# Seventeen instead of nine products of the identity with itself ahead of the first expert slot

## The chip, the cores and the metric

One core of one Trainium2 chip runs the whole program. The metric is the device time of one execution in microseconds (us), as the median of several runs. The kernel before takes 744.62 us (three runs, 742.53 to 746.62).

## The reference

The program computes three stages after one another, for a batch of 4 sequences of 576 tokens.

1. Attention with 8 heads of 64 columns, causal, with a bias that is made from a running sum of `s`.
2. A layer of 8 experts (512 to 1024 to 512 columns). Each token goes to one expert. The expert is the largest of 8 gate logits, or the expert of the token before where a local gate is high. The token's row is `relu(x @ w1[e]) @ w2[e]`, weighted by the softmax of the gate at `e`.
3. A dense layer: `h = relu(x @ w_in)`, a convolution of three taps along the tokens, a sigmoid gate, and `(h * gate) @ w_out`.

```python
for b in range(B):
    for s in range(S):
        fresh_e = argmax(logits[b, s])
        e = fresh_e if (s == 0 or local_gate[b, s] < 0.5) else prev_e
        h = maximum(x[b, s] @ w1[e], 0.0)
        out[b, s] = p[e] * (h @ w2[e])
```

## The kernel before, in words

The kernel is written by hand, engine by engine; the order of each engine's instructions is the order of the code, and semaphores join them. TensorE's program is attention, then `tensor_route`, `tensor_experts` and `tensor_block`. Nothing plans or reorders the work.

**Routing** (`tensor_route`, L1007 to L1038). VectorE finds each token's expert and its place in a list sorted by expert. The list is cut in 25 slots of 128 tokens, each slot belonging to one expert. TensorE helps with transposes, counts and sums. Between its waits it runs `keep_running` (L25 to L28): products of the 128x128 identity with itself, written to a PSUM bank that nobody reads. Each call of `matmul` there with float32 operands shows in the profile as two weight loads and two MATMUL rows, so nine products are 18 pairs. The last sum of routing gives the tokens of slots 8 to 24 (L1028, second part). Then comes the transpose of the convolution's weights (L1037), then nine products (L1038, shown as L28). After them begins `tensor_experts`.

**Experts** (`tensor_experts`, L1325 on). TensorE first waits for `slot_ready`, which VectorE gives with `slot_i` (L1141), the small table that says which half of the weight ring a slot uses and how many weight pieces must be there. `weights_of` reads two of its values into TensorE's registers (L1347 and L1348). Then `turn_first_x` (L1335 to L1340) waits for slot 0's tokens, which POOL's indirect DMA gathers from `x_rows` into `x_slots` (L1179), and turns them with four transposes. Two more products follow (L1411, shown as L28). VectorE takes the turned tokens to SBUF as a high and a low part (L1454, L1456). `hidden(0, (0,))` is 12 matmuls (L1365) for the first half of the hidden row. Then come `turn_x(1)` (L1331), the second half of `hidden(0)`, `turn_h(0)` (L1404), `turn_x(2)`, `hidden(1)`, `output(0)` (L1382), `turn_h(1)`, and so on. After slot 2 the pattern per slot is four transposes of tokens, 24 matmuls of L1365 and 24 of L1382.

**The other engines there.** VectorE, in order: the moves of slot 0's tokens, two low parts of expert 1's second matrix (L1530, semaphore `second_low`), the move of slot 1 (L1462, L1464), the moves of slot 0's hidden row (L1505, L1509), the tokens' weights (L1167 to L1174), and the two halves of `relu(1)` (L1496). POOL gathers slots 0 to 7, waits for `second_low`, writes `counted` (L1312), and gathers slots 8 to 24. ScalarE does the relu of slot 0 (L1296). SyncE's queue has nothing to issue there until VectorE hands over the first output row (L1260).

Of the kernel before, what the change touches and what calls it, by code (L numbers as in the profile page):

```python
# [24 lines left out]
def keep_running(nc, bank, identity, times):  # L25

    for _ in range(times):
        nc.tensor.matmul(bank[:, 0:P], identity[:, :], identity[:, :], start=True, stop=True)  # L28
# [744 lines left out]
def mixture(nc, ctx, sems, region, identity, attend, x_rows, y_sorted, w_gate, w_local, w1, w2, w_in, conv_w, w_out, out, h_turn):  # L773
# [89 lines left out]
    wide_bank = [sems.enter_context(nc.psum_tensor(f"wide_bank{n}", [P, 2, 512], F32)) for n in range(2)]  # L863
# [143 lines left out]
    def tensor_route(pe):  # L1007
        keep_running(nc, bank[1], identity, 9)
        pe.wait_ge(code_ready, 2)
        nc.tensor.transpose(wide_bank[0][0:T, 0, 0:P], small["rank_code"][:, :], identity[:, :]).then_inc(code_turned, 1)  # L1010
        keep_running(nc, bank[1], identity, 4)
        pe.wait_ge(seq_ready, 1)
        nc.tensor.matmul(bank[0][:, T:2 * T], expert_seq[:, P - 1:P].to_broadcast([T, P]), identity[0:T, 0:T], start=True, stop=True)
        nc.tensor.transpose(bank[0][:, 0:T], expert_seq[:, :], identity[0:T, 0:T]).then_inc(expert_turned, 1)
        flat_oh = oh[:, :, :].rearrange("p e t -> p (e t)")
        keep_running(nc, bank[1], identity, 4)
        pe.wait_ge(onehot_ready, 1)
        nc.tensor.matmul(wide_bank[1][:, 1, 0:E * T], all_ones[:, :], flat_oh, start=True, stop=True).then_inc(ranked, 1)
        nc.tensor.matmul(wide_bank[1][:, 0, 0:E * T], tri_less[:, :], flat_oh, start=True, stop=True).then_inc(ranked, 1)
        keep_running(nc, bank[1], identity, 15)  # L1020
        for part, slots in enumerate(SLOT_PARTS):
            pe.wait_ge(slot_tokens_ready, part + 1)
            for t in range(T):
                if t in BY_VECTOR:
                    pe.wait_ge(row_ready, t + 1)
                else:
                    pe.wait_ge(last_rows_ready, (t - BY_SCALAR[0]) // 3 + 1)
                last = nc.tensor.matmul((bank[1], row_bank[1])[part][:, 0:slots.stop - slots.start], row_is[:, t, :], slot_token[:, t, slots],  # L1028
                                        start=t == 0, stop=t == T - 1)

                if part == 0 and t % 3 == 1 and t < T - 1:
                    keep_running(nc, wide_bank[1][:, 0, :], identity, 1)
            last.then_inc(tokens_summed, 1)
            if part == 0:
                keep_running(nc, wide_bank[1][:, 0, :], identity, 6)
        pe.wait_ge(conv_loaded, 16)
        nc.tensor.transpose(row_bank[0][:, 0:K * KF], conv_nat[:, :], identity[0:K * KF, 0:K * KF]).then_inc(conv_turned, 1)  # L1037
        keep_running(nc, wide_bank[1][:, 0, :], identity, 9)  # L1038

    CHOICES = (slice(0, T - TB), slice(T - TB, T))  # L1040
    choice_steps = [0]
# [757 lines left out]
    def scalar_block(act):  # L1799
# [85 lines left out]
        for n in range(2):  # L1885
            act.wait_ge(out_stored[n], 16 * (NT // 2))

    return att, dict(sync=((sync_early, sync_between), sync_route, sync_experts), pool=(pool_early, pool_route, pool_experts, pool_block, first_low),
                tensor=(tensor_route, tensor_experts, tensor_block), vector=(vector_early, vector_route, vector_experts, vector_block, lambda dve: vector_choice(dve, 0)),
                scalar=(scalar_route, scalar_experts, scalar_block, first_high, load_gates))  # L1890

# [82 lines left out]
```

## Time and profile before

| what | us |
|---|---|
| median of three runs | 744.62 |
| profiled execution, whole | 744.3 |
| its span, first to last instruction | 742.6 |
| TensorE busy in the span | 720.5 (97%) |
| mean granted TensorE clock | 0.988 of full speed |

The span leaves out 1.7 us that lie around it. The granted clock has two levels in these profiles: 1.00 is 2.4 GHz and 0.50 is 1.2 GHz; a number between them is a stretch that holds both.

### The profile page before, as it was taken

The page shows a single profiled execution, that of the slowest core. Times are in us where ns is not written, and L with a number is a line of the kernel's source. Part 1 is how long each engine was busy: PE and PEld are TensorE (multiplying, and loading weights), DVE is VectorE, ACT ScalarE, POOL GpSimd, SP SyncE. Part 2 cuts the span into 40 slices and gives each one's busy share as a digit, 9 for nine tenths or more (in the row PEclk, how much of TensorE's full clock was granted, in tenths as well). Part 3 has the DMA queues.
Part 4 walks back from the last instruction along what each step waited for, and adds up shares of the span by engine and source line. Part 5 has one row for each costly group of instructions (what it writes and reads, how often), then busy time and mean ns, then how long its engine had stood idle before and what let it go on. Part 6 is the DMA issues. An engine that isn't in the chain of part 4 may idle for free.

```text
span 742.6 us, 13519 instructions
## 1 busy us (share of the span) xinstructions
PE 720.5 (97%) x4227; PEld 591.8 (80%) x4227; DVE 458.7 (62%) x1088; ACT 316.1 (43%) x634; POOL 328.4 (44%) x442
## 2 busy tenths in 40 slices
PE   8999999999979599999999999999999999999998
PEld 6676767767678487888888888888899889889986
DVE  5777778778766355566575665666399445536610
ACT  5777878778430022221412223020488335436620
POOL 8759888898236334644637647240521100000000
PEclk9999999999999799999999999999999999999999
DMA  8988888784075548786768877641421110000011
GB/s 177 217 213 227 207 224 229 210 206 134 17 216 159 137 164 273 252 271 232 256 210 300 255 241 254 220 138 44 142 64 30 43 36 15 30 30 14 29 43 56
DMA packets 114966, 115.35 MB, mean 155 GB/s; under 512 B 63804, under 2 KB 84052, under 8 KB 114900
## 3 DMA queue, kind: packets, MB, share of 16 engines
q1 hardware_dynamic: 94372, 68.54, 32.5%
q10 hardware_dynamic: 17056, 34.69, 14.2%
q0 software_dynamic: 3472, 11.28, 5.6%
q8 instruction: 38, 0.62, 0.3%
q14 instruction: 28, 0.23, 0.1%
HBM read 87.14 MB, written 27.34 MB: 154 GB/s over the span
## 4 chain that ended last, share of the span: by engine, by line
PE 67%; DVE 2%; another core or an unknown queue 2%; issue 1%; DMA 1%; ACT 0%; DVEq 0%; POOLq 0%; ACTq 0%
PE wide_bank L1365 18%; PE wide_bank L1694 14%; PE row_bank L1733 13%; PE row_bank L1382 9%; PE bank L1382 9%; PE bank L1331 1%; PE bank L1663 1%; DMA x_slots<-x_rows,token_of 1%; PE wide_bank L1404 0%; PE bank L1683 0%; PE wide_bank L28 0%; PE bank L1340 0%; PE row_bank L1683 0%; DVE y_sb L1524 0%
## 5 line engine op out<-in xcount | busy, mean ns | idle before, releaser
L914 POOL TENSOR_TENSOR ring<-raw_w,ring 128x2048 fp32r<-128x2048 f32 x28 | 128.7, 4619 | 117.2 <-ACT ring L904 117.2
L904 ACT ACTIVATE ring<-raw_w 128x2048 fp32r<-128x2048 f32 x30 | 55.8, 1908 | 209.3 <-DMA raw_w<-in_moe_w_dram 174.7
L1694 PE MATMUL wide_bank<-x_tr,ring 128*128 128x288 f32 x768 | 107.7, 297 | 0.0
L1694 PEld LDWEIGHTS wide_bank<-x_tr,ring 128*128 128x128 f32 x768 | 103.2, 188 | 0.9
L1733 PE MATMUL row_bank<-ring,g_tr 128*128 128x512 f32 x432 | 100.2, 390 | 0.0
L690 ACT ACTIVATE prob<-score,row_min 128x128 f32<-128x128 f32 (+2 forms) x144 | 83.4, 580 | 38.5 <-PE turn_ps L362 25.6
L1733 PEld LDWEIGHTS row_bank<-ring,g_tr 128*128 128x128 f32 x432 | 80.4, 188 | 16.2
L1785 DVE SCALAR_TENSOR_TENSOR conv<-h_pad,conv_col,conv 128x576 f32<-128x576 f32 x64 | 52.3, 817 | 53.8 <-ACT conv L1846 52.5
L252 POOL TENSOR_SCALAR bias<-ncum_row,cum_col 128x128 f32<-128x128 f32 (+3 forms) x128 | 66.8, 532 | 36.4 <-DVE row_min L551 33.4
L551 DVE CUSTOM_DVE_ANT_0 score<-score_ps,bias 128x128 f32<-128x128 f32 (+2 forms) x144 | 69.2, 514 | 19.9 <-issue 13.6
L1365 PE MATMUL wide_bank<-ring,xs_tr 128*128 x312 | 78.0, 406 | 3.3 <-DVE xs_tr L1456 1.8
L1382 PE MATMUL row_bank<-ring,h_tr 128*128 x312 | 73.4, 390 | 0.1
L1365 PEld LDWEIGHTS wide_bank<-ring,xs_tr 128*128 128x128 f32 x312 | 59.7, 195 | 16.6 <-issue 4.1
L1382 PEld LDWEIGHTS row_bank<-ring,h_tr 128*128 128x128 f32 x312 | 58.4, 188 | 12.9 <-issue 0.9
L1365 PE MATMUL wide_bank<-ring,xs_other 128*128 x288 | 68.5, 393 | 0.0
L1365 PEld LDWEIGHTS wide_bank<-ring,xs_other 128*128 128x128 f32 x288 | 53.2, 188 | 10.6
L1636 POOL DMA_INDIRECT y_tok<-y_sorted,place_i x20 | 20.2, 1008 | 77.2 <-PE bank L1663 46.7
L362 PE MATMUL turn_ps<-identity,prob 128*128 128x128 f32 x320 | 50.1, 279 | 1.0 <-ACT rest_tr L708 0.6
L362 PEld LDWEIGHTS turn_ps<-identity,prob 128*128 128x128 f32 x320 | 36.4, 141 | 11.6 <-issue 5.0
L322 PE MATMUL score_ps<-k_tr,q_tr 64*128 64x128 f32 (+3 forms) x256 | 44.9, 469 | 0.1
L1382 PE MATMUL bank<-ring,h_tr_other 128*128 x192 | 44.8, 389 | 0.0
L1837 ACT ACTIVATE h_pad<-wide_bank 128x576 f32<-128x576 f32 x32 | 20.9, 653 | 55.7 <-PE wide_bank L1694 55.4
(254 smaller groups left out, 1127.7 us busy)
## 6 DMA issues: line engine op xcount, KB each, us to landing
raw_w<-in_moe_w_dram ACTq DMA_DIRECT2D x12, 2048.0 KB, 11.2
x_slots<-h_turn SPq DMA_DIRECT2D x84, 128.0 KB, 2.9
ncum_row<-cum_rows SPq DMA_DIRECT2D x15, 512.0 KB, 4.9
y_sorted<-y_sb SPq DMA_DIRECT2D x26, 256.0 KB, 3.0
raw_w<-in_moe_w_dram SPq DMA_DIRECT2D x12, 512.0 KB, 4.4
h_turn<-h_sb SPq DMA_DIRECT2D x11, 512.0 KB, 5.3
h_turn<-x_slots SPq DMA_DIRECT2D x10, 512.0 KB, 7.2
ncum_tail<-cum_rows SPq DMA_DIRECT2D x32, 144.0 KB, 4.4
```

The costliest lines, as they stand in the source:

```text
L252: return nc.gpsimd.tensor_scalar(out, row, col, 1.0, ALU.add, ALU.mult)
L322: nc.tensor.matmul(out[:, hh, 0:(i + 1) * P], q_tr[u][at, i * P:(i + 1) * P], k_tr[u][at, 0:(i + 1) * P], start=True, stop=True).then_inc( ...
L362: last = nc.tensor.transpose(bank[:, at + j * P:at + (j + 1) * P], prob[unit(p, n) % 4][:, j * P:(j + 1) * P], identity[:, :])
L551: nc.vector.tensor_tensor_reduce(out=o, in0=a, in1=b, scale=1.0, scalar=3.0e38, op0=ALU.add, op1=ALU.min, accum_out=row_min[:, at % 4:at % ...
L690: nc.scalar.activation(prob[at % 4][:, 0:w], score[at % 3][:, 0:w], ACT.Exp, bias=row_min[:, at % 4:at % 4 + 1], scale=-1.0, accum_out=row ...
L904: nc.scalar.activation(high, whole, ACT.Copy).then_inc(high_ready, 1)
L914: nc.gpsimd.tensor_tensor(low, whole, high.bitcast(F32), ALU.subtract).then_inc(low_ready, 1)
L1365: last = nc.tensor.matmul(h_bank[:, half, :], xs_both[s % 2][:, a, kb, :], ring[:, bass.ds(n, 1), b, at:at + FH].rearrange("p a c -> p (a ...
L1382: last = nc.tensor.matmul(y_banks[s % 2][:, :], ht_of(s)[:, a, kb, :], ring[:, bass.ds(n, 1), 2 + b, kb * D:(kb + 1) * D].rearrange("p a c ...
L1694: last = nc.tensor.matmul(wide_bank[j % 2][:, half, 0:HALF], ring[:, 0, w, col:col + P], x2_tr[:, x, kb, at:at + HALF], start=kb == 0 and ...
L1733: last = nc.tensor.matmul(row_bank[outs % 2][:, :], g_tr[:, a, kb, lo:hi], ring[:, 0, 2 + w, kb * D:(kb + 1) * D], start=kb == 0 and (a, w ...
L1785: ins = V.scalar_tensor_tensor(c[:, :], h[:, k:k + S], conv_col[:, k * KF + f:k * KF + f + 1], c[:, :], ALU.mult, ALU.add)
```

## The change

One number: the last call of `keep_running` in `tensor_route` makes seventeen products in place of nine. It writes to the same PSUM bank, waits for nothing and gives no semaphore.

```diff
         pe.wait_ge(conv_loaded, 16)
         nc.tensor.transpose(row_bank[0][:, 0:K * KF], conv_nat[:, :], identity[0:K * KF, 0:K * KF]).then_inc(conv_turned, 1)
-        keep_running(nc, wide_bank[1][:, 0, :], identity, 9)
+        keep_running(nc, wide_bank[1][:, 0, :], identity, 17)
```

## Rows read from the trace of the kernel before

**Rows 1.** The page: busy time, clock in 40 slices, shares of the last chain.
```profile
PE 720.5 (97%) x4227; PEld 591.8 (80%) x4227; DVE 458.7 (62%) x1088; ACT 316.1 (43%) x634; POOL 328.4 (44%) x442
...
PEclk9999999999999799999999999999999999999999
...
PE 67%; DVE 2%; another core or an unknown queue 2%; issue 1%; DMA 1%; ACT 0%; DVEq 0%; POOLq 0%; ACTq 0%
```

**Rows 2.** Chain of waits, 213 to 256 us: start, length, what.
```profile
214.34 4.19 DMA x_slots<-x_rows,token_of
218.53 1.17 issue
219.69 1.77 PE bank L1340 x2
...
222.52 4.60 PE wide_bank L1365 x12
...
227.56 2.79 PE wide_bank L1365 x12
...
232.11 6.26 PE wide_bank L1365 x24
...
238.51 11.21 another core or an unknown queue
```

**Rows 3.** Timeline of PE: start, length, instructions [idle time before].
```profile
206.33 3.51 PE L28 MATMUL bank<-identity 128*128 128x128 f32 x30
...
215.25 2.27 PE L28 MATMUL wide_bank<-identity 128*128 128x128 f32 x18
219.69 0.63 PE L1340 MATMUL bank<-identity,x_slots 128*128 128x128 f32 x4 [2.17 <-issue]
220.16 0.61 PE L28 MATMUL wide_bank<-identity 128*128 128x128 f32 x4
222.52 4.60 PE L1365 MATMUL wide_bank<-ring,xs_tr 128*128 x12 [1.75 <-DVE xs_tr L1456]
```

**Rows 4.** All matmuls of L28 into `wide_bank`: ns min/median/max, first and last start.
```profile
L28 PE MATMUL wide_bank<-identity x46: 275/275/377, 210.4 to 220.5; 128*128 128x128 f32 x46
```

**Rows 5.** The clock by stretches: us, busy by engine (instructions), PEclk, DMA share, GB/s.
```profile
219.60:222.80 3.20, 1.36 (x9) 1.20 (x10) 1.24 (x4) 0.65 (x1) 2.59 (x3) 1.00 0.75 210
222.80:226.20 3.40, 3.40 (x9) 2.67 (x9) 3.40 (x3) 0.00 (x0) 3.08 (x2) 0.50 0.47 146
```

**Rows 6.** Who gives `slot_i`, and when PE's sequencer reads it (214 to 222 us).
```profile
217.62 0.40 DVE L1141 CAST slot_i<-slot_f 1x75 int32<-1x75 f32 x1
...
L1347 PEldq TENSOR_LOAD <-slot_i x1: 487/487/487, 218.1 to 218.1; - x1
...
L1348 PEldq TENSOR_LOAD <-slot_i x1: 316/316/316, 218.9 to 218.9; - x1
```

**Rows 7.** Such a register load at 304.8; PE's weight loads of L1365 from then on.
```profile
L1347 PEldq TENSOR_LOAD <-slot_i x1: 298/298/298, 304.8 to 304.8; - x1
...
304.82:308.60 3.78, 3.15 (x17) 1.00 0.41 135
```

**Rows 8.** Timeline of DVE and POOL, 221 to 250 us.
```profile
223.08 4.49 DVE L1530 TENSOR_TENSOR ring<-raw_w,ring 128x2048 fp32r<-128x2048 f32 x2
227.59 0.69 DVE L1462 CAST xs_other<-bank 128x512 fp32r<-128x512 f32 x1
227.69 0.09 POOL L1312 MEMSET counted<- 1x1 f32 x1 [1.51 <-DVE ring L1530]
238.45 0.69 DVE L1496 TENSOR_SCALAR h_sb<-wide_bank 128x512 f32<-128x512 f32 x1 [2.71 <-PE wide_bank L1365]
249.03 0.95 POOL L1179 DMA_INDIRECT x_slots<-x_rows,token_of  x1 [0.31 <-issue]
249.74 0.69 DVE L1496 TENSOR_SCALAR h_sb<-wide_bank 128x512 f32<-128x512 f32 x1 [10.60 <-remote]
```

**Rows 9.** Timeline of PE beside them.
```profile
231.87 5.71 PE L1365 MATMUL wide_bank<-ring,xs_other 128*128 x24
237.42 5.61 PE L1382 MATMUL row_bank<-ring,h_tr 128*128 x24
```

**Rows 10.** DMA queues, 233 to 235 us: packets, MB, share.
```profile
q8 instruction: 1, 0.02, 3.0%
```

## The prediction

> **What bounds the kernel now.** I began with the page. TensorE (PE) is busy 97% of the span, and 67% of the chain that ended last is PE's; its clock is full in all slices but one near the first third, where the digit is 7 [rows 1]. So the kernel is worth what PE's time is worth, and this change can only act around that one slice. Then I read the chain of waits there. It goes from the gather of slot 0's tokens to PE's transposes, to 12 matmuls of the first half of slot 0, which take 4.60 us, and to the 12 of the second half, which take 2.79 us [rows 2]. The reader is to see that these are the same work at two speeds. The windows say why: the granted clock is 0.50 (1.2 GHz) from 222.8 to 226.2 us and 1.00 (2.4 GHz) on both sides [rows 5]. Before it fell, PE's timeline had two idle times close together: 2.17 us ahead of the transposes of slot 0 and 1.75 us ahead of the first matmuls of L1365 [rows 3]. The change fills the first of them.
>
> Behind that the chain holds a piece of 11.21 us that is put down to nobody the profile knows [rows 2]. VectorE (DVE) does the first half of relu(1) at 238.45 and the second at 249.74, with 10.60 us idle between them, ended by "remote" [rows 8]. By the records the 24 matmuls that both halves wait for ended at 231.87 + 5.71 = 237.58 [rows 9], so TensorE's word to VectorE came some 12.1 us late. What holds it decides how much of any gain ahead of it survives.
>
> **The eight products.** They add 16 pairs of weight load and matmul to 18. How fast such pairs go: 30 take 3.51 us and 18 take 2.27 us [rows 3], and a single matmul of them 0.275 us [rows 4]. So a pair follows the one before by (3.51 - 0.275)/29 = 0.112 or by (2.27 - 0.275)/17 = 0.117 us. I take 0.112, from the longer run. Sixteen cost 1.8 us (up to 1.87), and the products end at 217.52 + 1.8 = 219.3 us (219.4 by the other). The transposes begin at 219.69. So all the added work lies in the idle time of 2.17 us, with 0.3 to 0.5 us to spare: cost on the path nothing. Without the cover they would cost the whole 1.8 us.
>
> **Can the products delay what PE's sequencer does?** The idle time is not the gather's alone. `slot_i` is given at 217.62 + 0.40 = 218.02, and the sequencer's two register loads begin at 218.1 and 218.9 and take 0.487 and 0.316 us, with some steps of their own behind each [rows 6]; the chain's 1.17 us of "issue" from 218.53 to 219.69 [rows 2] is the rest of this. The loads stand behind the products in the program, so the question is how far ahead of the array the sequencer gets. At 304.8 us it made such a load while 17 weight loads of the matmuls ahead of it overlap the stretch to 308.60, that is one under way and 16 still to come [rows 7]. With a lead of 16 pairs it can pass the new 34 when 18 have begun, at about 215.25 + 17 x 0.112 = 217.2 us. That is 0.9 us before `slot_i` comes. So the loads still begin at 218.1. A register load beside a busy array took 0.298 us at 304.8, less than the 0.487 here, so I count 0, with bounds of -0.2 (the first load at 0.298) and +0.3 us (array freed late and loads stretched as far as the spare time is short).
>
> **The clock.** What can be gained is the price of the low stretch: 4.60 - 2.79 = 1.81 us in the first 12 matmuls [rows 2]. The bounds are 0 (the clock falls as before: the 1.75 us idle and 0.3 us of the other stay, and just before the fall, from 219.6 to 222.8, PE was busy 1.36 us, on which the change has no hold [rows 3, 5]) and 1.81 us. I take the 1.81: the two idle times sum to 3.92 us now and to some 2.1 us with the change, and the other clock digits of the first third, with PE at 97% over the whole, are all 9 [rows 1].
>
> **What is late next.** With the first half done at 225.3 in place of 227.1, slot 1's transposes are 1.8 us earlier, but VectorE works on the two low parts until 227.57 and moves slot 1's tokens at 227.59 as before [rows 8]. That is no loss: PE has the second half of slot 0 to do until 228.6, and then slot 0's transposes. `hidden(1)` begins at about 230.1 and ends at 235.8 in place of 237.6, and `output(0)` follows it. VectorE's part of this shifts with it. POOL's doesn't: its gathers of slots 8 to 24 start from the end of L1530 (227.57, `counted` at 227.69), which hangs on the transposes of slot 0 and not on the matmuls behind them; they go on until 249.03 + 0.95 = 249.98 [rows 8]. The late word comes at 249.7, at the last gather's issue. So I read the hold as tied to the gathers and ending with them. Then the 1.8 us are swallowed: PE is idle 1.8 us longer before 250.49 and the rest of the kernel is where it was. The sum: 744.3 (profiled execution) + 0 (products) + 0 (register loads) - 1.8 (clock) + 1.8 (longer wait for the late word) = 744.3 us. The median of the runs shown is 0.3 above that execution, well inside their own spread of 4.1 us.
>
> The reading of the hold rests on a coincidence of two times only. The Trainium skill (Perfetto Trace Analysis, Tensor Engine Instruction) says that a matmul's end in the profile is estimated from its size, and that its semaphore goes out only once PSUM has acknowledged the writes. The 12.1 us between recorded end and release [rows 8, 9] agree with that. By this rule part of the hold could be TensorE's own unfinished work, which would start and end 1.8 us earlier: the sum would be 742.5 in place of 744.3.
>
> **The rivals.**
>
> *Carried through (742.5 us).* The hold keeps its length, 11.2 us, and so starts and ends 1.8 us earlier. For it: what is held is TensorE's, and TensorE is what moves. Against: it ends with POOL's gathers, whose DMAs keep their place. 744.3 - 1.8 = 742.5.
>
> *The clock falls anyway (744.3 us).* The change then doesn't do what it seems to be for. For it: the 3.2 us right before the fall look the same after the change [rows 5]. Against: 1.8 us less idle time altogether. Time as before.
>
> *The transposes' word comes sooner too (741.2 us).* The chain gives the first two transposes 1.77 us [rows 2], while all four take 0.63 [rows 3]; the first pair's word is thus about 1.3 us late, after an idle time of 2.17. If a PE that has just been busy gives it in time, VectorE, L1530 and the gathers all shift by 1.3 us, and with the clock it makes 3.1: 744.3 - 3.1 = 741.2. Against: gathers fill the DMA queues at that place as well, and they stay.
>
> *A longer hold (747.9 us, slower).* The place is TensorE's word after `hidden(1)`. It now falls at about 235.8, deeper inside the gathers. The first half's word was already late (L1496 at 238.45 for matmuls that were half done at about 234.8 [rows 8, 9]). If the change puts such a delay, 3.6 us, on the release that now comes at 249.7, the second half of relu(1) starts at 253.3 and the time is 744.3 + 3.6 = 747.9. It decides as soon as that release comes later than 249.7, since PE is idle by then. What could do it is also that 32 instructions more move every later block of PE's program: one block arrives between 233 and 235 us [rows 10], just before the first late word. The Trainium skill (Runtime: NRT & Kernel Launch, Instruction fetch mechanics) says that crossing a block of 256 instructions is mostly hidden; no run here prices it.
>
> **How the numbers follow.** Swallowed 0.40, falls anyway 0.17 (the same time, so 0.57 for 744.3), carried 0.25, the transposes' word too 0.10, longer hold 0.08. The likeliest time is 744.3. A measurement of this kernel can tell about 0.5%, 3.7 us, from no change. Around each case I put the spread of the runs, about 2 us to either side. Faster by over 0.5% is under 740.9: a bit less than half of the 741.2 case, and a tail of the carried one, and what shortens the hold itself, together 0.11. Slower by over 0.5% is over 748.3: nearly half of the longer hold and tails, 0.06. Within it 0.83. The range leaves out 2 in 10: from 741.3, which takes in the carried case with its spread, to 746.4.
>
> **What would show each step.** Right: PE's row of L28 from 215.25 has 34 instructions and ends by 219.4; the first register load is still at 218.1 and the transposes at 219.7; the 12 matmuls at 222.5 take about 2.8 us with the clock at 1.00; and VectorE's L1496 pair is still split, the second half at 249.7. Wrong: a register load that begins later than 218.3 (a lead shorter than 16 pairs), a clock of 0.50 after 222.8, the second L1496 at 247.9 (carried), transposes whose word comes by 220.2 (the gathers then shift too), or a release well after 249.7. The forecast as a whole is wrong if the time leaves 740.9 to 748.3.

## The result, and the profile after

The changed kernel is slower where it was first timed: 750.64 us median of 13 runs (748.57 to 755.03) against 746.99 us for the kernel before in 13 runs of the same series (742.53 to 754.05). The ratio is 1.0055, with a 95% interval of 1.0031 to 1.0078. The forecast was 744.3 us in a range of 741.3 to 746.4. Ratios are worked out over the single runs, without the few that lie over 1.5% above the fastest of their kernel, and so differ by up to 0.3% from the quotient of two medians.

Below, "word" is short for a semaphore that TensorE (PE) raises when a matmul has ended and that another engine waits for. A "pair" is one weight load and its MATMUL. The "lag" of slot 0 is the time from the start of its four transposes (L1340) to the start of VectorE's first move of them (L1454). Where words are on time it is 0.45 us.

First the timeline of the kernel after, PE and VectorE (DVE) and POOL together, for [rows 3, 8, 9]; columns as there.

```profile
215.84 4.06 PE L28 MATMUL wide_bank<-identity 128*128 128x128 f32 x34
218.02 0.19 DVE L1141 CAST slot_i<-slot_f 1x75 int32<-1x75 f32 x1
219.88 0.63 PE L1340 MATMUL bank<-identity,x_slots 128*128 128x128 f32 x4
220.34 0.61 PE L28 MATMUL wide_bank<-identity 128*128 128x128 f32 x4
223.93 0.95 POOL L1179 DMA_INDIRECT x_slots<-x_rows,token_of  x1 [0.30 <-issue]
226.39 0.42 DVE L1454 CAST xs_tr<-bank 128x256 fp32r<-128x256 f32 x1 [8.10 <-remote]
227.42 5.48 PE L1365 MATMUL wide_bank<-ring,xs_tr 128*128 x12 [6.47 <-DVE xs_tr L1456]
227.98 4.48 DVE L1530 TENSOR_TENSOR ring<-raw_w,ring 128x2048 fp32r<-128x2048 f32 x2
232.58 0.09 POOL L1312 MEMSET counted<- 1x1 f32 x1 [7.71 <-DVE ring L1530]
233.30 0.94 POOL L1179 DMA_INDIRECT x_slots<-x_rows,token_of  x1 [0.63 <-issue]
237.81 5.72 PE L1365 MATMUL wide_bank<-ring,xs_other 128*128 x24
243.36 3.79 PE L1382 MATMUL row_bank<-ring,h_tr 128*128 x16
247.39 0.39 PE L1382 MATMUL row_bank<-ring,h_tr 128*128 x1 [0.24 <-issue]
250.30 0.69 DVE L1496 TENSOR_SCALAR h_sb<-wide_bank 128x512 f32<-128x512 f32 x1 [8.62 <-remote]
253.32 0.94 POOL L1179 DMA_INDIRECT x_slots<-x_rows,token_of  x1 [0.30 <-issue]
257.33 0.69 DVE L1496 TENSOR_SCALAR h_sb<-wide_bank 128x512 f32<-128x512 f32 x1 [6.34 <-remote]
```

The two lines of the trace of before that go with them:

```profile
221.49 0.42 DVE L1454 CAST xs_tr<-bank 128x256 fp32r<-128x256 f32 x1 [3.47 <-PE bank L1340]
...
228.41 0.94 POOL L1179 DMA_INDIRECT x_slots<-x_rows,token_of  x1 [0.63 <-issue]
```

Read it from the top. The 34 pairs end at 219.90 and the transposes of slot 0 follow at once; the idle time of 2.17 us is gone, as intended. But VectorE's move of these transposes (L1454) starts 6.51 us after their start, where it was 1.80 us (221.49 - 219.69 [rows 3]). Its idle time is ended by "remote", which is what the profile writes here in place of the engine that gives the word. So PE is idle for 6.47 us in place of 1.75 ahead of L1365. VectorE's two low parts (L1530) and with them POOL's ninth gather move from 223.08 and 228.41 to 227.98 and 233.30, 4.9 us later. The second half of relu(1) moves from 249.74 [rows 8] to 257.33, 7.6 us later.

The chain of waits for [rows 2] has the two speeds of slot 0's matmuls again, and the piece put down to nobody now stands in front of them:

```profile
218.29 8.07 another core or an unknown queue
226.39 0.44 DVE xs_tr L1454
...
227.42 5.48 PE wide_bank L1365 x12
...
233.48 2.80 PE wide_bank L1365 x12
```

The windows for [rows 5] (us, busy by engine, PEclk, DMA share, GB/s):

```profile
219.60:222.83 3.23, 1.35 (x11) 1.02 (x9) 0.00 (x0) 0.83 (x1) 2.31 (x4) 1.00 0.73 217
222.83:233.07 10.24, 5.65 (x14) 4.41 (x15) 6.00 (x6) 0.13 (x1) 1.83 (x3) 0.50 0.27 84
```

The clock falls at the same time (222.8), now inside an idle time that lasts 6.47 us, and stays at its lower level for 10.2 us in place of 3.4. And the register loads for [rows 6]:

```profile
L1347 PEldq TENSOR_LOAD <-slot_i x1: 481/481/481, 218.2 to 218.2; - x1
...
L1348 PEldq TENSOR_LOAD <-slot_i x1: 319/319/319, 219.1 to 219.1; - x1
```

The span goes from 742.6 to 748.7 us, 6.1 us; the medians differ by 3.7 us. The traced execution of before was one of its shorter ones. How the 7.6 us at the second half of relu(1) come about: the transposes start 0.2 us later, their word comes 4.7 us later still, the first 12 matmuls take 0.9 us more, 0.2 us go elsewhere, and the word of hidden(1) comes 13.8 us after the recorded end of its matmuls (257.33 - 243.53) in place of 12.2, which is 1.6 us more.

### The profile page after: what moved, and what is told of

The parts are those of the page before. It is cut to its first block, busy times and chain, and to the rows that moved or that the text cites. A ratio compares the mean times of both kernels' runs of the same rounds, so it can differ in the third digit from the quotient of the medians.

```text
span 748.7 us, 13551 instructions
## 1 busy us (share of the span) xinstructions
PE 724.1 (97%) x4243; PEld 594.3 (79%) x4243; DVE 458.1 (61%) x1088; ACT 316.2 (42%) x634; POOL 326.8 (44%) x442
## 4 chain that ended last, share of the span: by engine, by line
PE 65%; DVE 3%; DMA 2%; issue 2%; another core or an unknown queue 1%; SPq 0%; ACT 0%; DVEq 0%; ACTq 0%
PE wide_bank L1365 17%; PE wide_bank L1694 14%; PE row_bank L1733 13%; PE row_bank L1382 9%; PE bank L1382 8%; PE bank L1331 1%; DMA y_sorted<-y_sb 1%; DMA h_turn<-h_sb 1%; PE bank L1663 1%; PE wide_bank L1404 1%; PE bank L1683 0%; PE wide_bank L28 0%; SPq L1254 0%; PE row_bank L1683 0%
## 5 line engine op out<-in xcount | busy, mean ns | idle before, releaser
L1365 PE MATMUL wide_bank<-ring,xs_tr 128*128 x312 | 77.3, 403 | 7.7 <-DVE xs_tr L1456 6.5
L1382 PE MATMUL row_bank<-ring,h_tr 128*128 x312 | 75.7, 394 | 7.0 <-issue 6.8
L1382 PEld LDWEIGHTS row_bank<-ring,h_tr 128*128 128x128 f32 x312 | 58.9, 189 | 21.1 <-issue 9.2
L1365 PEld LDWEIGHTS wide_bank<-ring,xs_tr 128*128 128x128 f32 x312 | 59.2, 193 | 20.4 <-issue 8.4
L1365 PE MATMUL wide_bank<-ring,xs_other 128*128 x288 | 68.8, 394 | 0.0
L1365 PEld LDWEIGHTS wide_bank<-ring,xs_other 128*128 128x128 f32 x288 | 53.2, 188 | 10.8
L1382 PE MATMUL bank<-ring,h_tr_other 128*128 x192 | 45.0, 390 | 0.5 <-DVE h_tr_other L1482 0.5
```

Source lines behind the costliest of these rows:

```text
L1365: last = nc.tensor.matmul(h_bank[:, half, :], xs_both[s % 2][:, a, kb, :], ring[:, bass.ds(n, 1), b, at:at + FH].rearrange("p a c -> p (a ...
L1382: last = nc.tensor.matmul(y_banks[s % 2][:, :], ht_of(s)[:, a, kb, :], ring[:, bass.ds(n, 1), 2 + b, kb * D:(kb + 1) * D].rearrange("p a c ...
```

## The experiments

**Theory A (backlog).** While POOL's gathers run, TensorE's words come out late, and the more instructions stand ahead of a word since the gathers began, the later. The eight products are 16 pairs more ahead of the word for slot 0's transposes. As first put, the theory said this of every chip; after the runs on chip 9 it was narrowed to chips with late words, and the runs on chip 3 tested the narrowed form.

**Rivals.** B: the 32 added instructions move the blocks in which PE's program is fetched. C: the time that the array works is what holds the words. D: idle time makes them late. E: the hold has a length of its own. F: the first trace was a chance.

The runs fell on several chips, and the chips proved to differ more than the kernels. I call them by numbers; the first comparison's chip has none. Ratios are to the kernel before on the same chip at the same time.

### Chip 8: where the instructions are, how many, and the gathers

`e1_shift`:

```diff
-        keep_running(nc, bank[1], identity, 4)
+        for _ in range(24):
+            nc.tensor.matmul(bank[1][:, 0:8], back[:, :], back[:, 0:8], start=True, stop=True)
         pe.wait_ge(seq_ready, 1)
```

> Nine products as before, but TensorE's program is 32 instructions longer ahead of them: the four products behind the transpose of the ranks (16 instructions) are replaced by 24 small float16 products (48 instructions) that take about as long. Theory A (backlog): while POOL's gathers run, TensorE's words come out late by an amount that grows with the number of instructions it has put behind them since the gathers began; nothing is added there, so VectorE's first L1454 starts about 1.8 us after the transposes of L1340 as before, and the time is that of before, within 2 us. Rival B (blocks): the change does harm because 32 instructions move the blocks of TensorE's program; then this kernel is slower by about 3.7 us like the changed one, with L1454 about 6.5 us after L1340.

Measured: ratio 0.9987 (0.9950 to 1.0025), lag 3.23 us:

```profile
219.27 0.63 PE L1341 MATMUL bank<-identity,x_slots 128*128 128x128 f32 x4 [2.28 <-issue]
222.50 0.42 DVE L1455 CAST xs_tr<-bank 128x256 fp32r<-128x256 f32 x1 [5.00 <-remote]
```

The instructions were moved by as much as in the change and nothing of 3.7 us came of it: rival B falls. The lag is not the 1.8 us that theory A expected. The kernel before was not traced on this chip; on chip 3 it later had 3.28 us, so 3.23 is probably what nine products give, and not an effect of the moved blocks.

`e2_wide`:

```diff
+def keep_wide(nc, bank, identity, times):
+
+    wide = identity[:, :].unsqueeze(1).to_broadcast([P, 4, P])
+    for _ in range(times):
+        nc.tensor.matmul(bank[:, :].rearrange("p (a c) -> p a c", a=4), identity[:, :], wide, start=True, stop=True)
 ...
-        keep_running(nc, wide_bank[1][:, 0, :], identity, 9)
+        keep_wide(nc, wide_bank[1][:, 0, :], identity, 4)
```

> In place of the nine products, four products of the identity with four copies of it side by side (512 columns): the array is busy for about 3.7 us as with seventeen, but with 8 pairs of weight load and matmul in place of 34 (18 before). Theory A (backlog of instructions): fewer instructions than before, so VectorE's L1454 starts no later than 1.8 us after L1340, the clock stays full after it, and the time is 0 to 3 us below before. Rival C (busy array): it is the time that the array spends on products, or PSUM's writes, that hold the words; then L1454 comes some 6 us after L1340 and the kernel is slower by about 3.7 us.

Measured: ratio 0.9975 (0.9934 to 1.0016). PE and VectorE in its timeline (L35 are the wide products, L1347 and L1461 are L1340 and L1454 of the kernel before):

```profile
214.53 3.70 PE L35 MATMUL wide_bank<-identity 128*128 128x512 f32 x8
218.99 0.63 PE L1347 MATMUL bank<-identity,x_slots 128*128 128x128 f32 x4 [0.76 <-issue]
219.44 0.43 DVE L1461 CAST xs_tr<-bank 128x256 fp32r<-128x256 f32 x1 [2.13 <-PE bank L1347]
```

The array works 3.70 us on products, nearly the 4.06 of the changed kernel, and the word is 0.45 us after the transposes. It is not the array's time: rival C falls.

`e3_none` leaves the call with nine products out.

> The call with nine products is left out. Theory A: the fewest instructions behind which the word of slot 0's transposes stands, so L1454 starts within 1 us after L1340; the clock falls around 222 us all the same (two idle times), at 1.8 us as before or a little more; time 0 to 2 us below before. Rival C expects the same. Rival D (it is the idle time that makes words late): L1454 would come later than 1.8 us after L1340 and the kernel would be slower.

Measured: ratio 0.9979 (0.9939 to 1.0020), lag 0.70 us, after 4.40 us of idle time ahead of the transposes. Rival D falls. The clock fell as early as 219.0 and the transposes themselves ran at the lower level (1.09 us for the four in place of 0.63).

```profile
219.39 1.09 PE L1339 MATMUL bank<-identity,x_slots 128*128 128x128 f32 x4 [4.40 <-issue]
220.09 0.42 DVE L1453 CAST xs_tr<-bank 128x256 fp32r<-128x256 f32 x1 [2.39 <-issue]
```

`e4_later`, with seventeen products:

```diff
-        gather_slots(pool, 4, 8)
-
         pool.wait_ge(second_low, PIECES // 2)
         nc.gpsimd.memset(counted[:, :], 0.0).then_inc(low_ready, PIECES // 2)
+        gather_slots(pool, 4, 8)
         pool.wait_ge(tokens_sorted, 2)
```

> Seventeen products, and POOL gathers slots 4 to 7 only after VectorE's two low parts (behind the memset of counted), so that only four gathers run beside slot 0's transposes. Theory A (backlog under gathers): with the gathers' traffic over by about 220 us, the word comes out by then, L1454 starts by 221.5 and the 12 matmuls behind it at full clock; the first stretch is 5 to 6 us shorter than in the changed kernel, and the gathers behind it last 5 us longer. Whole time: 1 to 4 us below the changed kernel, so within 2.5 us of before. A theory that leaves the gathers out (B or C) expects the changed kernel's time, 3.7 us above before, and L1454 about 6.5 us after L1340.

Measured: ratio 0.9984 (0.9941 to 1.0028). Its timeline:

```profile
214.68 4.06 PE L28 MATMUL wide_bank<-identity 128*128 128x128 f32 x34
219.12 0.63 PE L1339 MATMUL bank<-identity,x_slots 128*128 128x128 f32 x4 [0.39 <-issue]
219.81 0.42 DVE L1453 CAST xs_tr<-bank 128x256 fp32r<-128x256 f32 x1 [2.36 <-PE bank L1339]
220.84 3.01 PE L1364 MATMUL wide_bank<-ring,xs_tr 128*128 x12 [0.64 <-DVE xs_tr L1455]
```

The same 34 pairs are ahead of the transposes, with four gathers in place of eight, and the lag is 0.69 us in place of 6.5. The first 12 matmuls run at full clock, which is what the eight products were expected to bring. The changed kernel itself was not run on this chip, so the 6.5 us are those of the first comparison. The gain at slot 0 did not carry through to the next late word: the second half of relu(1) starts at 252.28, which is 18.0 us after the recorded end of its matmuls (228.60 + 5.71 = 234.31), the longest of all traces.

```profile
252.28 0.69 DVE L1495 TENSOR_SCALAR h_sb<-wide_bank 128x512 f32<-128x512 f32 x1 [17.69 <-remote]
```

### Chip 9: no late words

The next eight runs came to a chip on which the kernel before takes 731 us. Here are the kernel before and the changed one again, unedited, and the spreading of the gathers (`e5_spread`; `e6_spread17` is the same with seventeen products):

```diff
-        gather_slots(pool, 8, SLOTS)
+        gather_slots(pool, 8, 10)
         low_parts(pool, 2, 0)
         for e in range(2, E):
+            gather_slots(pool, min(10 + 4 * (e - 2), SLOTS), min(12 + 4 * (e - 2), SLOTS))
             low_parts(pool, e + 1, 0)
+            gather_slots(pool, min(12 + 4 * (e - 2), SLOTS), min(14 + 4 * (e - 2), SLOTS))
             low_parts(pool, e, 1)
```

> The kernel before once more, as the measure of how far a single trace and a single chip can be trusted. Ratio 1.00 within 0.3%. Theory A (backlog under gathers) expects that VectorE's L1454 starts 1.5 to 3.5 us after L1340 here as in the two traces with nine products so far (1.8 and 3.2), and that the held word of hidden(1) comes 0 to 7 us after the last gather is issued.

> The changed kernel once more on this chip. Theory A: L1454 starts 5 us or more after L1340, the ninth gather 4 us or more later than in the kernel before on this chip, and the time 2 to 5 us above it. If L1454 comes within 3.5 us here, the first trace of it was a chance and theory A loses its ground.

> Nine products. POOL gathers slots 0 to 9 as before and the other fifteen two at a time between its low parts, so that 15 dense gathers of 1.25 us each are no longer there while TensorE works on slots 0 to 2. Theory A: the long hold of hidden(1) (10.6 us) goes but for that of the first two gathers, so the time is 8 to 13 us below before. Theory E (the hold has its own length, whatever POOL does): as before, within 2 us. Either way POOL's low parts must still be in time; if they are late, TensorE waits for low_ready ahead of a slot and the gain shrinks.

> The same spreading with seventeen products. Theory A: the second hold goes, but eight gathers still run beside slot 0's transposes, so L1454 starts 5 us or more after L1340 and nothing behind it swallows that: 4 to 6 us slower than the spread kernel with nine products. Theory E: the changed kernel's time, some 3 us above before.

Measured: the kernel before against itself 0.9994 (0.9977 to 1.0011); changed 0.9976 (0.9950 to 1.0002); spread 1.0057 (1.0035 to 1.0079, five runs); spread with seventeen 1.0009 (0.9980 to 1.0039). None of the expectations that speak of lags of 1.5 us or more could be met, because the words are on time: the lag is 0.44 to 0.45 us in all four. By the expectation for the changed kernel (a lag under 3.5 us here, and theory A loses its ground) the theory as first put failed on this chip: gathers and 34 pairs alone do not make words late. PE and VectorE in the kernel before, then in the changed one:

```profile
218.48 0.63 PE L1340 MATMUL bank<-identity,x_slots 128*128 128x128 f32 x4 [1.76 <-DMA x_slots<-x_rows,token_of]
218.93 0.42 DVE L1454 CAST xs_tr<-bank 128x256 fp32r<-128x256 f32 x1 [2.04 <-PE bank L1340]
219.96 4.61 PE L1365 MATMUL wide_bank<-ring,xs_tr 128*128 x12 [0.40 <-DVE xs_tr L1456]
235.05 0.69 DVE L1496 TENSOR_SCALAR h_sb<-wide_bank 128x512 f32<-128x512 f32 x1 [1.26 <-PE wide_bank L1365]
```

```profile
218.85 0.63 PE L1340 MATMUL bank<-identity,x_slots 128*128 128x128 f32 x4
219.29 0.42 DVE L1454 CAST xs_tr<-bank 128x256 fp32r<-128x256 f32 x1 [2.04 <-PE bank L1340]
220.32 3.02 PE L1365 MATMUL wide_bank<-ring,xs_tr 128*128 x12 [0.40 <-DVE xs_tr L1456]
233.81 0.69 DVE L1496 TENSOR_SCALAR h_sb<-wide_bank 128x512 f32<-128x512 f32 x1 [1.26 <-PE wide_bank L1365]
```

Here the change does what its step of the prediction says: 4.61 us become 3.02, the clock stays full, and L1496 is 1.2 us earlier. One trace of each does not show it alone, since the spread kernel with nine products ran the same 12 matmuls in 3.01 us. The mean granted clock of the single runs does: over both series on this chip it is 0.999 or more in 14 of 20 of the changed kernel and in 2 of 57 of the kernel before. The spreading costs 4 us on this chip, where theory A had expected 8 to 13 us of gain. A later trace of it has PE waiting for VectorE's parts of the hidden row (L1482 in the kernel before) twice further on, for 1.4 and 2.2 us; I did not trace that cost to its cause.

Four more on the same chip. `e8_thirteen` has 13 in place of 9 in L1038; the others are the changed kernel, the wide products and the spread gathers again.

> The changed kernel again, since the chips differ: on the chip of the last four runs the kernel before takes 731 us and TensorE's words are never late. Where the kernel before takes 745 us or more (a chip with late words), theory A (backlog under gathers) expects L1454 5 us or more after L1340 and a ratio of 1.002 to 1.008; where it takes some 731 us, L1454 0.45 us after L1340, the 12 matmuls behind it at full clock, and a ratio of 0.9975 (1.81 of 731 us).

> Thirteen products, 26 pairs. With late words: L1454 2 to 6 us after L1340, between nine and seventeen; time between them. Without: L1454 at 0.45 us, the clock falls in some executions, ratio 0.998 to 1.000.

> Four products of 512 columns in place of nine of 128, again. Theory A with late words: L1454 within 1 us of L1340, the ninth gather by 227 us, ratio 0.990 to 0.999 and at least 0.4% below the changed kernel on this chip. Without late words: as the changed kernel, ratio 0.9975, since the array is as busy.

> Nine products, the gathers of slots 10 to 24 spread two by two between POOL's low parts, again. On a chip with late words theory A expects the words of hidden(1) to come within 4 us of the records, in place of 12, and a ratio of 0.985 to 0.993; theory E (a hold of its own length) expects 1.00. Without late words: 1.0057 as on the last chip, since nothing is gained and something behind it costs 4 us.

Measured: changed 0.9995 (0.9976 to 1.0014), thirteen 1.0032 (1.0011 to 1.0053, six runs), wide 1.0041 (1.0012 to 1.0070), spread 1.0066 (1.0049 to 1.0083, four runs). All lags are 0.45 us, and in all four the first 12 matmuls took the time of the full clock, in the spread kernel too, which has nine products and the idle time of 2.17 us:

```profile
220.46 0.63 PE L1342 MATMUL bank<-identity,x_slots 128*128 128x128 f32 x4 [2.17 <-issue]
...
221.94 3.01 PE L1367 MATMUL wide_bank<-ring,xs_tr 128*128 x12 [0.40 <-DVE xs_tr L1458]
```

So with nine products the clock at this place falls in some executions and not in others. The expectation for thirteen (0.998 to 1.000) and for wide (0.9975) missed: both traces have PE waiting for VectorE's L1482 further on, for 1.4 us in one and for 4.1 us in three waits in the other, which the changed kernel's trace has not. So a gain at slot 0 of 1 to 2 us is of the size of what the later pipeline gives and takes on this chip.

### Chip 3: late words again, three kernels side by side

> The changed kernel on one chip with the next two. Where the kernel before takes 745 us or more: theory A expects L1454 5 us or more after L1340 and the time 2 to 5 us above before; rival F (the first trace was a chance, words are late by some 0.5 to 6 us whatever the number of instructions) expects a lag no different from the two others' and a ratio of 0.998 to 1.001. Where it takes 731 us: 0.9975 to 0.9995.

> The kernel before, traced beside it. With late words: theory A expects L1454 1.5 to 3.5 us after L1340; rival F anything from 0.5 to 6. Ratio 1.00.

> Four products of 512 columns, 8 pairs of instructions. With late words: theory A expects L1454 within 1 us of L1340, as on the chip before last (0.45 us), and a time below both others; rival C (array time) expects f1's lag. Without late words: 0.45 us, ratio 0.998 to 1.004.

Measured: changed 1.0042 (1.0013 to 1.0071), 751.38 us; before against itself 1.0000 (0.9962 to 1.0038), 748.79 us; wide 0.9965 (0.9928 to 1.0002), 747.18 us. The word for slot 0's transposes, changed kernel, kernel before, wide products:

```profile
219.36 0.63 PE L1340 MATMUL bank<-identity,x_slots 128*128 128x128 f32 x4
226.00 0.42 DVE L1454 CAST xs_tr<-bank 128x256 fp32r<-128x256 f32 x1 [8.23 <-remote]
257.03 0.69 DVE L1496 TENSOR_SCALAR h_sb<-wide_bank 128x512 f32<-128x512 f32 x1 [13.40 <-remote]
```

```profile
218.89 0.63 PE L1340 MATMUL bank<-identity,x_slots 128*128 128x128 f32 x4 [2.19 <-issue]
222.17 0.42 DVE L1454 CAST xs_tr<-bank 128x256 fp32r<-128x256 f32 x1 [4.96 <-remote]
246.91 0.69 DVE L1496 TENSOR_SCALAR h_sb<-wide_bank 128x512 f32<-128x512 f32 x1 [9.26 <-remote]
```

```profile
218.62 0.63 PE L1347 MATMUL bank<-identity,x_slots 128*128 128x128 f32 x4 [0.35 <-issue]
219.06 0.42 DVE L1461 CAST xs_tr<-bank 128x256 fp32r<-128x256 f32 x1 [2.04 <-PE bank L1347]
```

Lags of 6.64, 3.28 and 0.45 us with 34, 18 and 8 pairs on one chip. The changed kernel's lag and its ratio came out as in the first comparison, so rival F falls. All traces from chips with late words together. The last column is the time from the recorded end of hidden(1)'s matmuls to the second half of relu(1):

| pairs in L1038's place | gathers beside them | lag of L1454, us | chip | late word of hidden(1), us |
|---|---|---|---|---|
| 0 | 8 | 0.70 | 8 | 15.6 |
| 8 (wide) | 8 | 0.45, 0.45 | 8, 3 | 2.9, 12.6 |
| 18 | 8 | 1.80, 3.23, 3.28 | first, 8, 3 | 12.2, 15.2, 8.4 |
| 34 | 8 | 6.51, 6.64 | first, 3 | 13.8, 15.2 |
| 34 | 4 | 0.69 | 8 | 18.0 |

The lag of slot 0 goes up with the pairs from 8 to 34, and with half the gathers it is gone. (The transposes of the row with 0 pairs ran at the lower clock and took 0.5 us longer.) The late word of hidden(1) follows neither number in these single traces. In the wide kernel with 2.9 us the long wait comes one word later: VectorE waits 12.3 us for that of `output(0)`. So the experiments account for the lag of slot 0, and not for the hold behind it, which also enters the whole time.

### Chip 5: the last three

> Nine products, gathers of slots 10 to 24 spread two by two between POOL's low parts. Where the kernel before takes 745 us or more: theory A (words held while gathers run) expects the second half of relu(1) within 4 us of its matmuls' recorded end (8.8 to 15.9 us in all traces with late words so far), and a ratio of 0.983 to 0.993; theory E (a hold of its own length) 1.00. Where it takes 731 us: 1.006.

> Seventeen products, gathers of slots 4 to 7 behind VectorE's low parts. With late words: theory A expects L1454 within 1.5 us of L1340 (0.69 once), against 6.5 us in the changed kernel, and a ratio of 0.996 to 1.001. If the gathers have no part, L1454 comes 6 us after L1340 and the ratio is 1.004. Without late words: 0.998 to 1.002.

> The wide products together with the spread gathers, a version meant to beat both kernels on a chip with late words: L1454 0.45 us after L1340, hidden(1)'s word within 4 us; ratio 0.98 to 0.99 there by theory A, 1.004 to 1.01 on a chip without late words, where spreading and the wide products each cost 3 to 4 us in waits for VectorE's L1482 further on.

Measured, on a chip without late words again (before 730.81 us): spread 1.0066 (1.0042 to 1.0091), seventeen with later gathers 0.9980 (0.9949 to 1.0011), wide and spread together 1.0042 (1.0010 to 1.0073). Lags 0.44 to 0.45 us. These bear out the parts of the expectations for such a chip and tell nothing of the rest. The first expectation's "8.8 to 15.9 us in all traces with late words so far" does not fit the table above, where they lie between 2.9 and 18.0. The spreading was thus never run where words are late, and what holds the word of hidden(1) stays open, rival E with it.

No version is shown to beat both kernels. The wide products are the best where words are late (0.9965 and 0.9975, both intervals reaching just past 1) and lose 0.4% on chip 9, where they are not. Seventeen products with later gathers read 0.9984 and 0.9980, one on each sort of chip, and neither interval leaves out 1.

Two things were not tested. What of the gathers counts, their traffic, their issue on POOL or something else, was not taken apart. And every execution timed here was recorded by the profiler (each has its span and clock), with a record for each weight load and each matmul, so what is recorded grows with the pairs as well. Whether the recording has a part in the late words is open.

## Why the prediction was wrong, point by point

**What bounds the kernel.** Right as far as it went: the one slice, the two speeds, the two idle times and the 11.21 us put down to nobody. It was read from a chip with late words, and nothing in one trace tells that on another chip the same kernel has none of them and takes 731 us.

**The eight products: cost.** 34 pairs took 4.06 us, and 0.275 + 33 x 0.112 makes 3.97. They filled the idle time, with no time left over, where 0.3 to 0.5 us were forecast. Their own time cost the path nothing: the transposes start 1.67 us after the end of `slot_i`'s move in both traces (218.02 to 219.69, 218.21 to 219.88).

**The sequencer.** Right: the first register load came at 218.2 right behind VectorE's L1141, which ended at 218.21 in place of 218.02, and the transposes at 219.88.

**The step that failed: "cost on the path nothing".** It was right for the products' own time and wrong for what they do to the word behind them. The prediction asked whether the products hold up the array or the sequencer. It had the symptom in hand: the word for the first two transposes 1.3 us late, in the rival of 741.2 us, which supposed that a busier PE would give it sooner. The opposite holds where words are late: 16 pairs more made it 3.4 us later on chip 3 (6.64 - 3.28) and 4.7 us in the first comparison (6.51 - 1.80). Taken as a term of the sum, it stood at 0 and measured +3.4 to +4.7. Why PE gives words late on these chips stays open.

**The clock.** The term of -1.81 us was right only where words are on time: 4.61 to 3.02 us on chip 9, -1.6 us, and there only in those executions in which the clock would have fallen. In the first comparison the wait made PE idle for 6.5 us, the clock was low for 10.2 us in place of 3.4, and the 12 matmuls took 5.48 us in place of 4.60. On chip 3 they took 4.34 us in place of 4.87. The sign named for this, a clock of 0.50 after 222.8, came.

**What is late next.** The prediction said that POOL's gathers would not move, since they hang on slot 0's transposes and not on the matmuls. The dependence is right, but the premise that slot 0's transposes give their word as before was not: the transposes' word moved, and the ninth gather with it, by 4.9 us (2.5 on chip 3). So the term of +1.8 us ("longer wait for the late word") failed too: nothing was swallowed, and the late word moved with the delay ahead of it, by 7.6 us. Its reading that the hold of hidden(1) ends with the last gather was a coincidence of the first trace: the second half of relu(1) starts 0.7 us after the last gather is issued there, 4.0 us after it in both traces of the changed kernel, and 4.1 us ahead of it in the kernel before on chip 3 (246.91 against 251.04).

The Trainium skill (Perfetto Trace Analysis, Tensor Engine Instruction) was weighed for the rule that a matmul's recorded end is an estimate and its semaphore follows the acknowledged write. The traces agree so far as that recorded end and word part by up to 18.0 us (`e4_later`: the matmuls of hidden(1) end by the record at 234.31, the second half of relu(1) starts at 252.28), and only on some chips. Whether PSUM's acknowledgement is what was late, they do not show.

**The rivals.** The longer hold at 747.9 us was nearest in sign and size, at a chance of 0.08, but it had another place: the word of hidden(1), not that of the transposes. That its time is near the one measured is luck. One of its means, the moved blocks of PE's program, is what `e1_shift` took away. On a chip without late words nothing is held, and the gain at slot 0 reaches hidden(1) (L1496 1.2 us earlier), as "carried through" has it.

**The range.** It was built on the profiled execution of 744.3 us; thirteen runs of the kernel before gave a median of 746.99, so 2.7 us of the miss of 6.3 are the starting point and 3.7 the change. The piece at 238.51 was bounded by one trace, and the range left it 2 us.

## What to carry to other kernels

Work that fills an idle engine is not free if another engine waits for something behind it: look at how late the words behind the idle time already are (the next engine's start against the recorded end), and take a lag there as a warning, not as slack. When an array must be kept busy, try few large instructions in place of many small ones: 8 pairs kept it busy for 3.7 us with a lag of 0.45 us, 34 pairs for 4.06 us with 6.6. It is no gain everywhere: on chip 9 the wide products were 0.4% slower. Before a change of 0.2% is judged, run the unchanged kernel on more than one chip: here chips differ by 2.1 to 2.6% on the same program, and the change costs 0.4 to 0.55% where words are late and nothing on chip 9 (0.9976 and 0.9995, neither interval leaving out 1).

## What the runs showed of the hardware that was not expected

- The same kernel takes 731 us on two chips (9 and 5) and 747 to 750 us on chips 8 and 3 and in the first comparison, whose chip may be one of these. The difference lies mostly in TensorE's words while POOL's indirect DMAs run: the second half of relu(1) starts at 249.74 in the first trace and at 235.05 on chip 9, 14.7 us apart, and the spans are 742.6 and 728.8. POOL issues one gather per 1.25 us on both sorts. Why the chips differ is not known.
- Where words are late, TensorE's own flow stops too. In the changed kernel's first trace, 12 + 4 + 4 + 4 + 24 + 16 = 64 pairs run at full pace from about the ninth gather's issue (233.3), and from 247.15 the matmuls of L1382 come one or two at a time, with idle times that end in "issue". The changed kernel's trace on chip 3 stops after 64 pairs as well, if half of the 12 matmuls at 231.57 are counted (6 + 8 + 4 + 24 + 22). In `e1_shift` the count is about 63, but in the first trace of the kernel before it is about 69 (7 + 4 + 4 + 4 + 24 + 24 + 2), so the number is not the same everywhere. A store of some fixed size that drains slowly under the gathers would look like this, and would also give lags that grow with the pairs. That is inferred from counts, not shown.
- TensorE's sequencer made its register loads with some 16 pairs still ahead of it [rows 7], in slot after slot: in the kernel before at 233.5, 275.2 and 304.8 us, where the 24 weight loads of L1365 had begun at 231.84, 273.52 and 303.28 and follow each other by 0.22 us, so that some 8 had begun and 16 were to come.
